# Reordered queues in an attention and feed-forward kernel: the first pair of heads, the last group, the gates and the last store

## The reference

```python
# batch 2, 8 heads, 768 positions, head width 64; all float32
q_bucket, k_bucket = 6 sign bits of q @ proj and of k @ proj
mask = q_bucket[:, :, :, None] == k_bucket[:, :, None, :]
scores = where(mask, scale * q @ k.T, -1e9)
attn = exp(scores - max) / (sum + 1e-9)
x = (attn @ v), heads side by side            # 1536 x 512
h = maximum(maximum(x @ w1, x @ w2), x @ w3)  # 1536 x 768
x = h @ w_out                                 # 1536 x 512
h = x @ w_in2                                 # 1536 x 2048
g = h / (1 + exp(-1.702 * h))
out = g @ w_out2                              # 1536 x 512
```

## Time and profile before

| what | before |
|---|---|
| median of 3 runs | 672.24 us (672.01 to 672.71) |
| profiled execution, its own time | 672.6 us |
| its span | 670.8 us |
| TensorE clock granted | 1.00 of full speed (2.4 GHz), all of the span |
| busy: PE, DVE, POOL, ACT | 663.7, 495.9, 474.2, 346.6 us |
| stages, from the span's start | first pair to 34 us; loop over groups to 222; last group and first products to 249; first feed-forward to 423; last stage to 667; stores to 671 |

### The profile page before, as it was taken

How to read it: one execution, slowest core, us unless ns; L and a number is a source line. 1 busy time by engine, 2 the same in 40 slices (tenths; PEclk the granted TensorE clock), 3 DMA queues, 4 the chain that set the end, 5 groups by cost and what they waited for, 6 DMA issues and landing times.

```text
span 670.8 us, 11966 instructions
## 1 busy us (share of the span) xinstructions
PE 663.7 (99%) x3892; PEld 576.8 (86%) x3892; DVE 495.9 (74%) x976; ACT 346.6 (52%) x761; POOL 474.2 (71%) x538
## 2 busy tenths in 40 slices
PE   8999999999999999999999999999999999999998
PEld 6776777777777699999999999988898988989896
DVE  6878878788788799869778963678877666555554
ACT  6887777877777630011103453555545554454433
POOL 6774756788876899968870528799987776777710
PEclk9999999999999999999999999999999999999999
DMA  6673836638352111111110201212232124212102
GB/s 159 152 161 102 192 88 155 151 88 187 91 132 75 34 32 32 32 32 33 32 40 25 95 1 33 79 48 80 79 93 64 64 78 143 64 64 65 45 18 94
DMA packets 58492, 54.17 MB, mean 81 GB/s; under 512 B 28640, under 2 KB 47488, under 8 KB 58432
## 3 DMA queue, kind: packets, MB, share of 16 engines
q1 hardware_dynamic: 56784, 53.02, 29.2%
q10 hardware_dynamic: 1648, 0.39, 0.3%
HBM read 32.51 MB, written 3.15 MB: 53 GB/s over the span
## 4 chain that ended last, share of the span: by engine, by line
PE 88%; POOL 6%; issue 2%; ACT 1%; DVE 1%; DMA 1%; DVEq 0%; ACTq 0%; POOLq 0%
PE psO L1544 10%; PE psS L1522 10%; PE psR L1530 9%; PE psR L1628 7%; PE psR L1627 7%; PE psR L1629 7%; PE psS L1627 6%; PE psS L1628 6%; PE psS L1629 6%; PE psS L1730 4%; PE psS L1729 4%; PE psS L1728 4%; POOL w_lo L736 3%; PE psR L1470 1%; POOL w_raw L727 1%
## 5 line engine op out<-in xcount | busy, mean ns | idle before, releaser
L577 POOL TENSOR_SCALAR probs<-probs,lone,inv 128x768 f32<-128x768 f32 x96 | 93.9, 985 | 58.6 <-DVE inv L1145 58.5
L736 POOL TENSOR_TENSOR w_lo<-w_raw,w_hi 128x256 fp32r<-128x256 f32 x96 | 79.2, 838 | 44.6 <-ACT w_hi L982 43.9
L1128 DVE TENSOR_REDUCE neg_max<-psS 128x1 f32<-128x768 f32 x96 | 91.2, 950 | 12.9 <-PE psS L1522 8.7
L803 ACT ACTIVATE probs<-psS,neg_max 128x768 f32<-128x768 f32 x96 | 86.5, 901 | 15.7 <-DVE neg_max L1128 15.6
L560 POOL TENSOR_SCALAR w_hi<-w_raw 128x256 fp32r<-128x256 f32 (+1 forms) x79 | 49.0, 624 | 50.2 <-PE psS L1629 28.9
L812 ACT ACTIVATE probs_t<-psR 128x384 f32<-128x384 f32 x131 | 60.7, 491 | 31.2 <-PE psR L1530 30.7
L1530 PE MATMUL psR<-ident,probs 128*128 128x128 f32 x576 | 74.6, 273 | 0.4 <-POOL probs L577 0.2
L1530 PEld LDWEIGHTS psR<-ident,probs 128*128 128x128 f32 x576 | 66.5, 140 | 5.5 <-POOL probs L577 2.1
L1544 PE MATMUL psO<-probs_t,v_raw 128*64 128x384 f32 x384 | 68.8, 494 | 0.0
L1379 DVE TENSOR_TENSOR v_raw<-psR,early 128x384 f32<-128x384 f32 x64 | 35.3, 552 | 32.4 <-PE psR L1629 32.2
L1384 DVE TENSOR_TENSOR v_raw<-v_raw,bits 128x384 f32<-128x384 f32 x64 | 53.7, 841 | 6.7 <-ACT bits L1005 4.3
(11 more groups left out here) (275 smaller groups left out, 1881.5 us busy)
## 6 DMA issues: line engine op xcount, KB each, us to landing
w_raw<-in_moe_w_in SPq DMA_DIRECT2D x16, 512.0 KB, 3.4
w_raw<-in_moe_w_out SPq DMA_DIRECT2D x32, 256.0 KB, 2.7
w_raw<-in_moe_w SPq DMA_DIRECT2D x9, 512.0 KB, 3.8
h_lo<-w_hi SPq DMA_DIRECT2D x22, 192.0 KB, 3.3
h_hi<-w_hi SPq DMA_DIRECT2D x18, 192.0 KB, 3.4
w_raw<-in_q SPq DMA_DIRECT2D x16, 192.0 KB, 3.6
v_raw<-in_v SPq DMA_DIRECT2D x16, 192.0 KB, 2.5
stacks<-w_hi SPq DMA_DIRECT2D x16, 192.0 KB, 3.3
```

Source lines behind the costliest of these rows:

```text
L577: pool.tensor_scalar(probs[i % PROBS][:, :], probs[i % PROBS][:, :], lone[:, i % 6:i % 6 + 1], inv[:, i % 6:i % 6 + 1], ALU.add, ALU.mult) ...
L736: pool.tensor_tensor(in2_slot(w_lo, n, which), in2_raw(n, PARTS2[which]), f32(in2_slot(w_hi, n, which)), ALU.subtract).then_inc(in2_split, 1)
L803: act.activation(probs[i % PROBS][:, :].rearrange("p (a b) -> p a b", a=2), psS[i % 2][:, :, 0:HALF], ACT.Exp, bias=neg_max[:, i % 6:i % 6 ...
L1128: dve.tensor_reduce(neg_max[:, i % 6:i % 6 + 1], psS[i % 2][:, :, 0:HALF], AX.XY, ALU.min).then_inc(max_ready, 1)
```

## The change

The order of instructions is changed, and nothing else: the same operations run on the same data.
- First pair, ScalarE: exponential 3 in front of copy (0,1), 6 in front of (2,0), 8 in front of (4,0) and (4,1), 10 in front of (6,1). TensorE: scores 8 in front of turning (3,1), scores 9 in front of (4,0) and (4,1), the first half of the values of unit 0 in front of (6,0) and (6,1). VectorE: `row_max(7)` in front of copy (2,1).
- Last group: TensorE does the values of unit 14 in front of the first three turnings. GpSimd's `first_block(3)` stands behind the last norm. VectorE does `invert_sums(95, 1)` in front of copy (93,0), and copy (95,1) in front of `x_lo_unit(14)`.
- Last stage: `EARLY_GATES` goes, its early order holds for every mix. In mix 2 `mix(2, 6)` stands in front of `g_lo(2, 1)`.
- End: the second half of the last store is issued by ScalarE instead of SyncE.

```diff
--- before.py
+++ after.py
@@ -75,8 +75,6 @@
     FIRST_MIX = {2 * OUTS * B - 4: (0,), 2 * OUTS * B - 3: (1, 2), 2 * OUTS * B - 2: (3, 4), 2 * OUTS * B - 1: (5, 6)}
 
     POOL_PARTS = 7 + 3
-
-    EARLY_GATES = 5
     T_ORDER = [(0, 1), (0, 2), (0, 3), (0, 4), (1, 1), (1, 3), (1, 2), (1, 4)]
     RING = 3
     MARKS = 2 * 6
@@ -539,10 +537,9 @@
                 if n == FPS2 + 1:
                     store_results(0)
             store_results(B - 1)
-            for h in range(2):
-                which, done = result_done(B - 1, LAST)
-                sync.wait_ge(which, done + h)
-                sync.dma_start(out_r[B - 1, :, LAST, ts(h, LAST_COLS)], result[LAST][:, ts(h, LAST_COLS)]).then_inc(stored, 16)
+            which, done = result_done(B - 1, LAST)
+            sync.wait_ge(which, done)
+            sync.dma_start(out_r[B - 1, :, LAST, ts(0, LAST_COLS)], result[LAST][:, ts(0, LAST_COLS)]).then_inc(stored, 16)
             sync.wait_ge(stored, 16 * (NT * B + 1))
 
 
@@ -681,8 +678,9 @@
                         for step in range(6 * (p - PAIRS // 2) + 3 * st - 6, 6 * (p - PAIRS // 2) + 3 * st - 3):
                             if step < 16:
                                 sums_of_x(step)
-                    if p == PAIRS - 1:
+                    if p == PAIRS - 1 and n < GROUPS - 1:
                         first_block(st)
+            first_block(3)
 
             for k in range(1, BLOCKS):
                 pool.wait_ge(w_loaded[k % 3], 16 * (k // 3 + 1))
@@ -853,27 +851,27 @@
             copy_qk(2, 1)
             exp_tile(2)
             copy_turned(0, 0)
+            exp_tile(3)
             copy_turned(0, 1)
-            exp_tile(3)
             copy_turned(1, 0)
             exp_tile(4)
             copy_qk(3, 0)
             exp_tile(5)
             copy_qk(3, 1)
             copy_turned(1, 1)
+            exp_tile(6)
             copy_turned(2, 0)
-            exp_tile(6)
             copy_turned(3, 0)
             copy_turned(3, 1)
             exp_tile(7)
+            exp_tile(8)
             copy_turned(4, 0)
             copy_turned(4, 1)
-            exp_tile(8)
             copy_turned(5, 0)
             copy_turned(5, 1)
             exp_tile(9)
+            exp_tile(10)
             copy_turned(6, 1)
-            exp_tile(10)
             copy_turned(7, 0)
             copy_turned(7, 1)
             copy_turned(8, 0)
@@ -1077,10 +1075,9 @@
                         in2_hi(n + 1, which)
                 out2_hi(2 * n)
                 out2_hi(2 * n + 1)
-                if n < EARLY_GATES:
-                    sigmoid(n, 0)
-                    g_hi(n, 0)
-                    sigmoid(n, 1)
+                sigmoid(n, 0)
+                g_hi(n, 0)
+                sigmoid(n, 1)
                 if n + 1 < MIXES:
                     in2_hi(n + 1, 5)
                     in2_hi(n + 1, 6)
@@ -1088,11 +1085,9 @@
                     y_sum_hi(1, T_ORDER2[n - 2])
                 if n + 2 < MIXES:
                     in2_hi(n + 2, 0)
-                for which in range(3):
-                    if n >= EARLY_GATES or which > 1:
-                        sigmoid(n, which)
-                    if n >= EARLY_GATES or which > 0:
-                        g_hi(n, which)
+                g_hi(n, 1)
+                sigmoid(n, 2)
+                g_hi(n, 2)
                 if n == FPS2:
                     copy_result(0, COPIES[0][0])
                     copy_result(0, COPIES[0][1])
@@ -1103,6 +1098,10 @@
             act.activation(result[LAST], acc[LAST], ACT.Copy).then_inc(last_begun, 1)
             for tile_ in COPIES[0]:
                 copy_result(B - 1, tile_)
+
+            which, done = result_done(B - 1, LAST)
+            act.wait_ge(which, done + 1)
+            act.dma_start(out_r[B - 1, :, LAST, ts(1, LAST_COLS)], result[LAST][:, ts(1, LAST_COLS)]).then_inc(stored, 16)
 
 
         @block.vector
@@ -1211,8 +1210,8 @@
             invert_sums(3, 2)
             row_max(6)
             invert_sums(5, 1)
+            row_max(7)
             copy_turned(2, 1)
-            row_max(7)
             row_max(8)
             make_bits(1)
             invert_sums(6, 2)
@@ -1227,8 +1226,11 @@
                 p, st = n // 4, n % 4
                 if n < GROUPS:
                     row_max(3 * n)
-                copy_turned(3 * n - 3, 0)
+                    copy_turned(3 * n - 3, 0)
                 invert_sums(3 * n - 1, 1)
+                if n == GROUPS:
+                    copy_turned(3 * n - 3, 0)
+                    copy_turned(3 * n - 1, 1)
                 if n < GROUPS:
                     row_max(3 * n + 1)
                     invert_sums(3 * n, 2)
@@ -1238,7 +1240,7 @@
                     x_lo_unit(n // 2 - 2)
                 if n < GROUPS:
                     row_max(3 * n + 2)
-                copy_turned(3 * n - 1, 1)
+                    copy_turned(3 * n - 1, 1)
 
             def t_add(n, o, one, two, op):
                 if n > 0:
@@ -1436,9 +1438,12 @@
                 g_lo(n, 0)
                 gate(n, 1)
                 mix(n, 5)
+                if n == 2:
+                    mix(n, 6)
                 g_lo(n, 1)
                 gate(n, 2)
-                mix(n, 6)
+                if n != 2:
+                    mix(n, 6)
                 g_lo(n, 2)
                 if n == FPS2:
                     copy_result(0, COPIES[1][0])
@@ -1579,19 +1584,19 @@
             scores(7)
             turn_probs(2, 1)
             turn_probs(3, 0)
+            scores(8)
             turn_probs(3, 1)
-            scores(8)
             project(1)
+            scores(9)
             turn_probs(4, 0)
             turn_probs(4, 1)
-            scores(9)
             turn_probs(5, 0)
             turn_probs(5, 1)
             scores(10)
+            for c in range(TH):
+                times_values(0, c)
             turn_probs(6, 0)
             turn_probs(6, 1)
-            for c in range(TH):
-                times_values(0, c)
             turn_probs(7, 0)
             scores(11)
             turn_probs(7, 1)
@@ -1602,13 +1607,16 @@
                 halves = [(i, j) for i in range(3 * n - 3, 3 * n) for j in range(2)]
                 if n < GROUPS:
                     scores(3 * n)
-                for i, j in halves[:3]:
-                    turn_probs(i, j)
-                if n < GROUPS:
+                    for i, j in halves[:3]:
+                        turn_probs(i, j)
                     scores(3 * n + 1)
                 u, part = (n - 3) // 2, (n - 3) % 2
                 for c in range(TH * part, TH * part + TH):
                     times_values(u, c)
+                if n == GROUPS:
+
+                    for i, j in halves[:3]:
+                        turn_probs(i, j)
                 if st < 2 and p + 1 < PAIRS:
                     turn_qk(2 * p + 2 + st)
                 if st == 2 and p + 1 < PAIRS:
```

## The result

The changed kernel takes 673.42 us (median of 21 runs, 672.96 to 673.87); the kernel before, run beside it, 672.15 (21 runs, 671.98 to 672.89). The ratio is 1.0016 [1.001, 1.0022], slower by 1.1 us where I forecast 0.6 us faster. (The two medians lie 1.27 apart: the times of before lie in two heaps, and its median falls in the lower one.) That is within the 0.2% I called "about the same", but outside my range. The profiled execution took 673.7 us, its span is 671.9.

A forecast was written before the change was run, and what follows sets the result against it. TensorE, busy 663.7 of 670.8 us, was taken as the bound, so only its gaps could be gained. +0.6 - 0.37 - 0.74 - 0.1 = -0.6 us against the median 672.24 gave 671.6 us; range 670.0 to 672.9.

The forecast's parts named there:

- the end of the attention: Last group: values fill TensorE's wait for the norms, but plain(1, 0) waits for the last x_lo: -0.37 us.
- mix 9: Last stage: sigmoid(9, 0) moved forward starts its gate about 1.1 us earlier and removes up2(9, 6)'s wait: -0.47 us.
- first pair: First pair of heads, until 34 us: the new order makes scores 12 later, +0.6 us, bounds +1.1 and -2.2.
- mix 2: Last stage at 457 us: mix(2, 6) in front of g_lo(2, 1) removes the wait of up2(3, 1): -0.27 us.
- the store: Last store: its second half issued from ScalarE goes some 0.2 us earlier, but DMA is full: -0.1 us.
- the step on which the forecast hung: First pair: ScalarE still has copy (3,1) in front of exponential 7, which starts at 25.36 instead of 24.65 us.
- the moved copies and x_lo_unit(14) start those sums no earlier (228.9 in either order): End of the attention: VectorE's row of sums starts at 228.9 us, before and after the change.
- a cap: End of the attention: plain(1, 0) needs the last x_lo, so TensorE comes at most 0.37 us earlier.
- the -0.48 I had: Last group: of 0.67 us lost in the transposes, 0.2 comes back through the three ring banks, leaving -0.48 us.
- the second rival: Last stage: early gates meet GpSimd's parts, up2(n + 1, 1) waits 0.27 in ten mixes; +2.6 us, 674.8; chance 0.09.
- the nothing that the sum has for early gates that meet GpSimd: Last stage, mixes from n = 5: the sum holds no loss for gates stretched by GpSimd's parts.
- TensorE's cover: Last stage: the 3.1 us TensorE gives mix(n, 6) behind its product before up2(n + 1, 1) must wait.

The follow-up runs named there:

- experiment 2: Kernel before with only the last group's new order (TensorE, VectorE's copies, GpSimd's first_block(3)): 672.40 us against 672.18, ratio 1.0004.
- experiment 5: Kernel before, unchanged, run for a second profile: 672.44 us against 672.12, ratio 1.0.
- Experiment 6: Kernel before with the changed first pair, but exponential 7 in front of copy (3,1): 672.00 us against 672.12, ratio 1.0.
- experiment 9: Kernel before with only ScalarE's and VectorE's new first-pair order, TensorE's order old: 672.43 us against 672.37, ratio 1.0003.
- experiment 12: As experiment 9, but exponential 6 back behind copy (2,0): 671.85 us against 672.13 for the kernel before, ratio 0.9994.
- experiment 10: Kernel before with the changed first pair, except scores 8 stay behind turning (3,1): 672.41 us against 672.37, ratio 1.0002.
- experiment 1: Kernel before with only the first pair's new order: 672.83 us against 672.18, ratio 1.001.
- experiment 3: Kernel before with only early gates in every mix and mix(2, 6) in front of g_lo(2, 1): 672.37 us against 672.18, ratio 1.0004.
- experiment 4: The whole change without the first pair's part, against the kernel before: 672.86 us against 672.18, ratio 1.0008.
- experiment 8: As experiment 3, but without early gates in mix 8: 672.25 us against 672.12 for the kernel before, ratio 1.0005.
- experiment 11: Kernel before with experiment 9's pair, last group's order with earlier last x_lo, early gates in mixes 0-4 and 9, mix(2, 6) early: 671.71 us against 672.37, ratio 0.9992.
- experiment 13: As experiment 11, but with the first pair of experiment 12: 671.15 us against 672.13 for the kernel before, ratio 0.9985.

## Why the prediction was wrong

**The sum, corrected.** Three terms failed: the end of the attention (-0.37 in the sum, +0.13 measured), mix 9 (-0.47, for a wait that an ordinary execution doesn't have) and mix 8 (not in the sum at all, +0.47). Against an ordinary execution of before, which has no gap in mix 9, the changed kernel is at first pair +0.67, end of the attention +0.13, +0.06 about 19 us behind `plain(1, 0)` (experiment 2), +0.06 in small steps up to mix 2 such as the unchanged kernel of experiment 5 has too, mix 2 -0.27, mix 8 +0.47, mix 9 nothing: +1.12. The ratio gives 0.0016 x 672.15 = 1.08 (0.67 to 1.48). Predicted was -0.6. Of the 1.7 between them 0.5 is mix 9, 0.47 mix 8, 0.5 the end of the attention, 0.1 the store and 0.2 small terms.

**The first pair: right.** Predicted +0.6, measured +0.58 at scores 12 by itself. The chain came as written, less the 0.43 by which this execution started later: exponential 7 at 25.32 (forecast 25.36), scores 9 at 26.36 (26.41), scores 10 at 28.62 (28.55), scores 12 at 34.26 (34.2). Also right was that VectorE doesn't reach `row_max(6)` earlier, because of what GpSimd holds. VectorE's timeline of the kernel after:

```profile
20.78 0.59 DVE L1135 TENSOR_SCALAR lone<-neg_max 128x2 f32<-128x2 f32 x1
...
22.00 0.94 DVE L1127 TENSOR_REDUCE neg_max<-psS 128x1 f32<-128x768 f32 x1
```

and GpSimd's:

```profile
19.50 1.84 POOL L570 TENSOR_TENSOR w_lo<-w_raw,w_hi 128x768 fp32r<-128x768 f32 x1
```

The two-column operation ends at 21.37, GpSimd's at 21.34, and the row maximum starts at 22.00 - 0.43 = 21.57 (forecast 21.56). The Trainium skill calls the ports that VectorE and GpSimd share an exclusive lock, which whoever issues first holds for the whole instruction when VectorE is in a two-port mode, as TENSOR_SCALAR can be (SBUF — State Buffer, section Who interferes with whom); the two ends, 0.03 us apart, agree. Experiment 6 confirms the step on which the forecast hung, copy (3,1) in front of exponential 7: without it the pair is 0.73 faster. What I had not seen is that TensorE's new order isn't the only fault. With TensorE's old order the pair still loses 0.21 (experiment 9), now because exponential 6 holds copy (2,0) back; with that one line undone it gains 0.46 (experiment 12). From there the loss can be added up in one order of steps: exponential 6 forward +0.67, scores 9 and the values forward +0.10 (experiment 10), scores 8 forward +0.31 (experiment 1), together from -0.46 to +0.62. The steps aren't independent, so these are not prices that hold in another order: in the pair as changed turning (3,1) comes behind scores 8 and doesn't wait for the ring bank at all. Whether exponential 6 costs anything there is open; the run that would show it is the changed pair with that one line undone.

**The end of the attention: the failed step is "the moved copies and x_lo_unit(14) start those sums no earlier (228.9 in either order)", and with it the -0.37.** It was a cap worked out for a row of sums that stays where it was. VectorE's timeline of the kernel after:

```profile
229.22 0.56 DVE L1151 COPY probs_t<-psR 128x384 f32<-128x384 f32 x1 [1.36 <-PE psR L1535]
229.70 0.55 DVE L1157 TENSOR_TENSOR x_lo<-psO,x_hi 128x384 fp32r<-128x384 f32 x1
230.16 0.98 DVE L1248 TENSOR_TENSOR probs<-x_hi,early 128x768 f32<-128x768 f32 x1
231.17 1.38 DVE L1248 TENSOR_TENSOR probs<-probs,x_lo 128x768 f32<-128x768 f32 x1
...
241.32 0.54 DVE L1157 TENSOR_TENSOR x_lo<-psO,x_hi 128x384 fp32r<-128x384 f32 x1
```

and of the kernel before, the first two sums:

```profile
228.89 1.11 DVE L1246 TENSOR_TENSOR probs<-x_hi,early 128x768 f32<-128x768 f32 x1
230.03 1.04 DVE L1246 TENSOR_TENSOR probs<-probs,x_lo 128x768 f32<-128x768 f32 x1
```

The copy of the last turning now stands in front of `x_lo_unit(14)`, so the two follow each other behind a turning that comes late, and the sums start at 230.16 - 0.43 - 0.67 = 229.06 instead of 228.89. The row itself takes 11.16 us (230.16 to 241.32) where it took 10.93 (228.89 to 239.82, the second time from the earlier trace rows); its second sum, for one, is 1.38 long, and before it was 1.04. So `x_lo(15)` is 0.40 later by VectorE's clock, not at the same place, and the gain of 0.29 is turned into a loss of 0.13, of which 0.10 is the slow first matmul behind the wait. The saving itself was also smaller than the -0.48 I had. TensorE's timeline of the kernel after:

```profile
226.72 2.46 PE L1535 MATMUL psR<-ident,probs 128*128 128x128 f32 x18
228.94 0.42 PE L1635 MATMUL psS<-x_hi,w_hi 128*128 128x384 f32 x1
```

The last 18 transposes take 2.22 us where I had 1.96 + 0.2, and the nine in front of the values 1.07 (223.56 to 224.63) where I had 0.98. Why the row of sums got longer is open: GpSimd's parts lie otherwise beside it, but GpSimd was busy beside it before as well, and no run isolates it.

**Mix 2: right** (-0.27 forecast; from the matmul in front of the gap to the second behind it -0.27 in experiments 3, 4, 8, 11, 13 and the kernel after).

**Mix 9: the failed step is the -0.47.** The rows were read rightly and show what happened in that execution. They don't show what happens in most. And the term was counted twice: I had set the profiled execution at 0.4 above the median and carried that over, when the gap of 0.47 was the reason for it (672.6 - 0.47 = 672.13, at the median of 672.15). One execution's wait, released by a gate stretched to 2.92 us where its own kind has a median of 0.75, asked for a second profile.

**Mix 8: the second rival, in one mix instead of ten.** The failed step is the nothing that the sum has for early gates that meet GpSimd. The rival's mechanism (GpSimd's parts beside the last gates) is the one seen, and TensorE's cover was enough in nine of the ten mixes. I had read the cover from `mix(n, 6)` and the product `up2(n + 1, 1)` alone. In mix 8 VectorE also copies the finished results of the first batch behind the last `g_lo`, and a bank that TensorE wants depends on it. The rival's 2.7 us was wrong in size, 0.47 is what it cost.

**The store: -0.1 forecast, nothing found.** The last matmul starts 3.56 us before the end of the span in both profiles. SyncE's and ScalarE's issues in the kernel after:

```profile
668.94 0.46 SPq L542 DMA_DIRECT2D out<-results  x1
```

and

```profile
669.15 0.36 ACTq L1104 DMA_DIRECT2D out<-results  x1
```

The second half is issued 0.21 us behind the first instead of 0.48, somewhat more than forecast. The DMA engines are full until the last bytes (the kernel after, the stretch of 666 to 671.9 in 40 slices), so it ends with the bytes:

```profile
DMA  0000299994899999999999999999999999200000
```

**What stays open.** Why scores 3 start anywhere from 15.23 to 15.94 us in sixteen profiles. Between the profile of before and that of experiment 5 nearly all of the 0.50 us arises in the first six transposes, which turn the first data loaded (behind them TensorE goes on at 5.80 in the one and at 6.25 in the other). The times of before lie in two heaps some 0.5 us apart (about 671.8 to 672.4 and 672.5 to 672.9), which this start would explain; those of the changed kernel don't part so clearly, and only three of the profiled executions are of one kernel. How often mix 9's gap occurs. What exponential 6 costs under TensorE's new order, why the row of sums got longer, and the 0.06 at about 260 us.

## What to carry to other kernels

When an operation is moved forward in a queue, ask first what it pushes back: in experiment 9 exponential 6 was wanted earlier and came earlier, but the 0.4 us copy that it overtook freed the next ring bank, and that decided. A wait of less than 1 us in one profile may belong to that execution alone; before it is priced, and above all before the profile's distance to the median is added to it, look whether a second profile has it. And when a gap is removed, follow the next wanted result back through its own queue with the new order: here the cap was right as a rule and wrong in place, because the change moved the cap as well.

## What the runs showed of the hardware

- The same 128x384 multiplication on VectorE, at the same place of the same program, took 2.92 us in one execution and 0.69 and 0.73 in two others. In the first it started 0.35 us behind the start of a GpSimd TENSOR_TENSOR of 256 columns and was held over that one and the next three; in the others it started 0.2 us in front of the same one.
- A two-column VectorE operation with one input was held 0.59 us here and 1.75 in the earlier trace rows, both times until a GpSimd TENSOR_TENSOR of 768 columns ended. So two columns don't protect an operation. One column does here: of the same two lines' one-column operations 24 start while such a GpSimd instruction runs in the kernel before, and none takes over 0.15 us.
- Behind a short wait the second matmul starts 0.27 us after the first instead of 0.17 (384 columns, 241.92 to 242.19), and 0.33 instead of 0.23 (512 columns, 552.07 to 552.40). The two waits, shown as 0.2 us, cost 0.45 and 0.47.
